# The first chunk's probabilities: transposed by products with a scaled diagonal instead of being scaled first

## Chip, cores and metric

One core of one Trainium2 chip. The metric is the device time of one execution in microseconds; beside it stands the span of the profiled execution, from its first to its last instruction. Lower is better.

## What is computed

Top-k attention followed by two feed-forward layers, all in fp32. There are 4 batches, 8 heads, 576 positions, head width 64, 2304 tokens in all; the feed-forward layers go 512 to 2048 to 512.

```python
scores = scale * np.matmul(q, k.transpose(0, 1, 3, 2))
kth = np.partition(scores, -top_k, axis=-1)[..., -top_k:-top_k + 1]      # top_k = 32
scores = np.where(scores >= kth, scores, -1000000000.0)
scores = scores - np.max(scores, axis=-1, keepdims=True)
attn = np.exp(scores)
attn = attn / (np.sum(attn, axis=-1, keepdims=True) + 1e-09)
out = np.matmul(attn, v)
...
x = out as [2304, 512]
x = max(0.01 * h, h) @ w_out,          h = x @ w_in      # first layer
x = curve(h) @ w2_out,                 h = x @ w2_in     # second layer
```

## The kernel before

**Items and tiles.** Attention is cut into 80 items (`ITEMS`). An item is up to 128 rows of one pair of heads: two tiles of 128 rows by 576 scores, one for each head (a few "mixed" items hold the last 64 rows of both heads in one tile). 144 tiles in all. Four head pairs with the same rows make a chunk's input: chunk 0 is batch 0, rows 0 to 255, that is items 0 to 7, tiles 0 to 15 (`starts_early(it.gp)` is true for just these). There are seven chunks (`CHUNKS`).

**Steps.** All engines follow one written-out order of steps s = 0, 1, 2, ..., each engine with its own in-order list of instructions and semaphores between them. `score_step` says in which step an item's scores are made, `exp_tile` which tile's exponential stands in a step, `out_step` when an item is transposed: items 0 to 7 go out in steps 6, 8, 10, ..., 20. `make_plan` fills the steps from 21 on (`READY[0]`) with units of the feed-forward layers; before step 21 there are none, apart from the first three units' products over three quarters of the input, which stand just ahead of item 7's transposes in step 20.

**An item's way.** TensorE makes the scores (L923, L924) in PSUM; ScalarE copies them scaled to SBUF (L1102, L1109). VectorE finds the 32 largest of each row with four MAX8 (L1304) and three MATCH_REPLACE8 (L1308) a tile, some 5 us a tile. ScalarE's `keep` (L1128, L1130) masks by the 32nd value, `exponential` (L1138) makes the probabilities in `probs` and their row sums. VectorE closes the sum (`close_sum`, L1315) and inverts it (`invert_sum`, L1320). Then `normalise` multiplies the probabilities by it, in place: the first head's 576 columns on ScalarE (L1144), the second head's on GpSimd (L798), for item 7 on VectorE (L1325). TensorE's `transpose` turns them in nine transposes with the identity (L939, L945, and L946 for the last 64 columns of both heads at once). ScalarE copies them to `p_t` and `p_rem` (`copy_transposed`, L1151, L1152), one step after the transposes. After two items of a head pair TensorE multiplies with the values (L962), ScalarE copies the result as the chunk's input (L1172, L1174), GpSimd makes its low half (L804).

**ScalarE's order in a step before 21**: `normalise` of the item that goes out, `copy_transposed` of the one before, `copy_values`, `keep`, score copies, `exponential`, weight pieces. **TensorE's**: scores, values, transposes, scores that are spilled.

**Spilled scores.** Items 22 to 27 get their scores in steps 7, 9, 11, 13, 17 and 18 (`SPILLED_AT`), long before their turn. ScalarE copies them into one of three stages (`stages`: the buffers `part_r`, `part_o` and `y_acc`, which are not yet in use), SyncE stores them to DRAM (L685) and loads them again later (L692). The first hidden unit (`read_bank`, `u.h == 0`) waits for the last store of each stage.

**Feed-forward.** A unit is 128 output rows of a layer's half: products with weights split in a high and a low part (L1003, L1004, L1011). Weights come through `raw`, are split by ScalarE (L1088, L1079) and GpSimd (L792, L785, L781).

Of the kernel before, what the change touches and what calls it, by code (L numbers as in the profile page):

```python
# [8 lines left out]
ALU = mybir.AluOpType  # L9
ACT = mybir.ActivationFunctionType  # L10

P = 128
B, H, S, D = 4, 8, 576, 64
# [6 lines left out]
KC = S // P  # L20
MAIN = KC * P
REST = S - MAIN
# [64 lines left out]
T_SLOTS = 4  # L87
# [128 lines left out]
def starts_early(gp):  # L216

    return gp <= CHUNKS[0].last_gp
# [29 lines left out]
FIRST_LATE = min(it.n for it in ITEMS if it.first > READY[0] + 2)  # L248
SPILLED_AT = {22: 7, 23: 9, 24: 11, 25: 13, 26: 17, 27: 18}
SPILLED = list(SPILLED_AT)  # L250
STAGES = 3


def score_step(it):
# [258 lines left out]
def by_pool(it):  # L513

    return it.gp <= CHUNKS[1].last_gp and not it.mixed and it.last != FIRST_END and not sooner(it)


def by_dve(it):
    return not it.mixed and not by_pool(it)


def scaled(kind, it):

    return sum(kind(o) for o in ITEMS[:it.n + 1])


def need(eng, sem, value):
    if value > 0:
        eng.wait_ge(sem, value)


def build(nc, kqd, vd, wd, out_t):
# [3 lines left out]
    with ExitStack() as ctx:  # L536
        def sb(name, shape, dt=F32):
            return ctx.enter_context(nc.sbuf_tensor(name, shape, dt))

        def ps(name, shape):  # L540
            return ctx.enter_context(nc.psum_tensor(name, shape, F32))

        def sem(name):
            return ctx.enter_context(nc.semaphore(name))
# [11 lines left out]
        row_inv = sb("row_inv", [P, T_SLOTS, 2])  # L556
# [3 lines left out]
        ident = sb("ident", [P, P])  # L560

        gate = sb("gate", [P, 2, GATE_COLS], F32R)
        part_r = sb("part_r", [P, G_SLOTS, WIDE])
        part_o = sb("part_o", [P, G_SLOTS, WIDE])
        y_acc = sb("y_acc", [P, CK, WIDE])
# [2 lines left out]

        raw = sb("raw", [P, RAW_SLOTS, PIECE])
        later = xy[:, 1, :, :, :].rearrange("p h c n -> p (h c n)")  # L570
        stages = [part_r[:, :, :].rearrange("p a n -> p (a n)"), part_o[:, :, :].rearrange("p a n -> p (a n)"),
                  y_acc[:, :, :].rearrange("p a n -> p (a n)")]
        stages = [a[:, 0:2 * S].rearrange("p (h n) -> p h n", h=2) for a in stages]
        split = later[:, 0:SPLIT_SLOTS * 2 * PIECE].rearrange("p (a h n) -> p a h n", a=SPLIT_SLOTS, h=2)

        ps_s = ps("ps_s", [P, 2, 512])
        ps_t = ps("ps_t", [P, 2 * KC, P])
        ps_av = ps("ps_av", [P, 512])
        ps_f = ps("ps_f", [P, BANKS, 512])
        ps_rem = ps_av[:, WIDTH:WIDTH + P]  # L580
# [11 lines left out]
        out_stored = sem("out_stored")  # L592
        spill_stored = [sem("spill_stored%d" % a) for a in range(STAGES)]
        spill_loaded = [sem("spill_loaded%d" % a) for a in range(S_SLOTS)]

        zeroed = sem("zeroed")
        ident_ready = sem("ident_ready")
# [11 lines left out]
        probs_ready = sem("probs_ready")  # L609
        probs_ready_pool = sem("probs_ready_pool")  # L610
        probs_ready_dve = sem("probs_ready_dve")
        transposed = sem("transposed")
# [19 lines left out]

        def spilled(it, where):
            return where[:, 0:it.tiles, :]

        def x_parts(gp):


            b, g = divmod(gp // PAIRS, 2)
            first = g * GROUP_WIDTH[0]  # L640
            buf, pair, width = xy[:, b % 2, :, :, :], gp % PAIRS, GROUP_WIDTH[g]
            if b < B - 1:
                spans = [(first, 0, width)]
            elif g == 0:
                spans = [(WIDE, 0, S - WIDE), (0, S - WIDE, width - S + WIDE)]
            else:
                spans = [(first + WIDE - S, 0, width)]
            return [(buf[:, 0, pair, to:to + n], buf[:, 1, pair, to:to + n], slice(at, at + n)) for to, at, n in spans]
# [22 lines left out]
        def _(sp):  # L671
# [10 lines left out]
            def store_spilled(it):  # L682
                a = SPILL_ORDER.index(it.n)
                sp.wait_ge(scores_copied, 2 * PLACE[it.n] + 2)
                sp.dma_start(spilled(it, s_dram[a, :, :, :]),  # L685
                             spilled(it, stages[a % STAGES])).then_inc(spill_stored[a % STAGES], 16)

            def load_spilled(it):
                a = SPILL_ORDER.index(it.n)
                sp.wait_ge(spill_stored[a % STAGES], 16 * (a // STAGES + 1))  # L690
                sp.wait_ge(kept, ITEMS[it.n - S_SLOTS].last + 1)
                sp.dma_start(spilled(it, scores[:, it.n % S_SLOTS, :, :]),  # L692
                             spilled(it, s_dram[a, :, :, :])).then_inc(spill_loaded[it.n % S_SLOTS], 16)
# [75 lines left out]
        def _(pool):  # L769
# [24 lines left out]

            def normalise(it):
                pool.wait_ge(inv_ready, it.n + 1)
                p = probs[:, it.n % P_SLOTS, S:2 * S]
                pool.tensor_tensor(p, p, row_inv[:, it.n % T_SLOTS, 1:2].to_broadcast([P, S]),  # L798
                                   ALU.mult).then_inc(probs_ready_pool, 1)
# [62 lines left out]
            for s, (first, second, third) in enumerate(PLAN):  # L862
                if s < READY[0] and s in OUT_AT and by_pool(OUT_AT[s]):
                    normalise(OUT_AT[s])
                if s >= READY[0] and s + 1 in OUT_AT and by_pool(OUT_AT[s + 1]):
                    normalise(OUT_AT[s + 1])
# [28 lines left out]
        def _(pe):  # L895
# [31 lines left out]
            def transpose(it):  # L927
                pe.wait_ge(probs_ready, it.n + 1)
                if by_pool(it):
                    pe.wait_ge(probs_ready_pool, scaled(by_pool, it))  # L930
                elif by_dve(it):
                    pe.wait_ge(probs_ready_dve, scaled(by_dve, it))
                if ITEMS_SCORED[it.n] > SCORED_EARLY:
                    pe.wait_ge(scores_copied, 2 * ITEMS_SCORED[it.n])
                need(pe, p_t_copied, it.n)
                need(pe, x_copied, it.gp)
                p = probs[:, it.n % P_SLOTS, :]
                for c in range(KC):
                    pe.transpose(ps_t[:, c, :], p[:, c * P:(c + 1) * P], ident[:, :])  # L939
                if it.mixed:  # L940
                    pe.transpose(ps_t[:, KC, :], p[:, S - P:S], ident[:, :])
                    pe.transpose(ps_rem[0:REST, :], p[:, MAIN:S], ident[:, :]).then_inc(transposed, 1)
                    return
                for c in range(KC):
                    pe.transpose(ps_t[:, KC + c, :], p[:, S + REST + c * P:S + REST + (c + 1) * P], ident[:, :])  # L945
                pe.transpose(ps_rem, p[:, MAIN:MAIN + P], ident[:, :]).then_inc(transposed, 1)  # L946
# [89 lines left out]
            for s, (first, second, third) in enumerate(PLAN):  # L1036
                if s < READY[0]:
                    for it in SCORED_AT[s]:
                        score(it)
                    if s - 1 in VALUES_AT:  # L1040
                        values(VALUES_AT[s - 1])
                    if s == READY[0] - 1:
                        pe.wait_ge(top_ready, FIRST_END + 1)
                        for u in EARLY_UNITS:
                            begin(u)
                    if s in OUT_AT:
                        transpose(OUT_AT[s])
                    for it in SPILL_AT[s]:
                        score(it)
                    if s == READY[0] - 1:  # L1050
                        values(VALUES_AT[s])
                    continue
# [12 lines left out]
                if s in OUT_AT:  # L1065
                    transpose(OUT_AT[s])
# [6 lines left out]
        def _(act):  # L1073
# [17 lines left out]
            def copy_scores(it):  # L1091
                k = PLACE[it.n]
                dst = scores[:, it.n % S_SLOTS, :, :]
                if it.n in SPILLED_AT:
                    a = SPILL_ORDER.index(it.n)
                    dst = stages[a % STAGES]
                    need(act, spill_stored[a % STAGES], 16 * (a // STAGES))
                if k == 0:
# [41 lines left out]

            def normalise(it):
                act.wait_ge(inv_ready, it.n + 1)
                p = probs[:, it.n % P_SLOTS, 0:S]
                act.activation(p, p, ACT.Copy, scale=row_inv[:, it.n % T_SLOTS, 0:1]).then_inc(probs_ready, 1)  # L1144

# [30 lines left out]
            def read_bank(u):  # L1176
# [13 lines left out]
                if u.h == 0:  # L1190
                    for a in range(min(STAGES, len(SPILLED))):
                        act.wait_ge(spill_stored[a], 16 * len(range(a, len(SPILLED), STAGES)))
# [37 lines left out]
            for s, (first, second, third) in enumerate(PLAN):  # L1230
# [41 lines left out]
                if done and sooner(done):  # L1272
                    normalise(done)
                if s + 1 in OUT_AT and not sooner(OUT_AT[s + 1]):
                    normalise(OUT_AT[s + 1])
# [20 lines left out]
        def _(dve):  # L1296
# [24 lines left out]

            def normalise(it):
                dve.wait_ge(inv_ready, it.n + 1)
                p = probs[:, it.n % P_SLOTS, S:2 * S]
                dve.tensor_scalar(p, p, row_inv[:, it.n % T_SLOTS, 1:2], None, ALU.mult).then_inc(probs_ready_dve, 1)  # L1325

# [62 lines left out]
            for s in range(-VECTOR_AHEAD, len(PLAN)):  # L1389
# [15 lines left out]
                if new:  # L1405
                    it = ITEM_OF[t]
# [104 lines left out]
```

## Time and profile before

| | |
|---|---|
| median of three runs | 1159.14 us (1154.64 to 1160.17) |
| profiled execution | 1157.35 us, its span 1155.5 us |
| TensorE, products | 1090.2 us busy (94%) |
| VectorE | 870.8 us (75%) |
| ScalarE | 779.5 us (67%) |
| GpSimd | 477.3 us (41%) |
| mean granted TensorE clock | 0.984 of full |

The busy shares are averages over a head, in which the first chunk's attention is made, a middle, in which attention and feed-forward run side by side, and a long rest. The profile says for each instruction when it started, how long it took, and what ended the idle time of its engine before it. The granted clock is 1.00 at 2.4 GHz and 0.50 at 1.2 GHz. A group of equal instructions in a row is merged into one line of the timeline (x4), and its duration includes the last one's tail.

### The profile page before, as it was taken

To read this page: it belongs to the slowest core of one execution; us is meant where nothing else is said; L and a number is where in the kernel's file an instruction comes from. 1 tells how busy PE (TensorE), PEld (TensorE's weight loads), DVE (VectorE), ACT (ScalarE), POOL (GpSimd) and SP (SyncE) were. 2 spreads that over 40 slices of the span, in tenths; PEclk is the share of its full clock that TensorE was granted. 3 is DMA by queue.
4 is the path that set the end of the run, shared out by engine and by line. 5 is a ranking of instruction groups with operands and counts; after the bars stand their busy time and mean duration, and the time that the engine had idled before them with its cause. 6 is when DMAs were issued, how large, how long until landed. Compare 5 with 4: busy or idle time off the path is not lost.

```text
span 1155.5 us, 21187 instructions
## 1 busy us (share of the span) xinstructions
PE 1090.2 (94%) x7544; PEld 1003.5 (87%) x7544; DVE 870.8 (75%) x1914; ACT 779.5 (67%) x1804; POOL 477.3 (41%) x514
## 2 busy tenths in 40 slices
PE   5467998999999999999999999999999999999998
PEld 3246887799989999999998879998899999999998
DVE  7999978999999898999979979988994005300234
ACT  6777879876698777887779858678785224322332
POOL 5864659552363332642236324134441134222322
PEclk9889999999999999999999989999999999999999
DMA  7998988988667787888766757656456577787774
GB/s 236 374 400 324 400 311 312 360 333 311 234 206 262 248 308 281 291 293 289 240 231 235 244 182 242 215 194 205 148 188 228 203 253 254 256 297 246 256 247 137
DMA packets 92407, 302.59 MB, mean 262 GB/s; under 512 B 10256, under 2 KB 13968, under 8 KB 92304
## 3 DMA queue, kind: packets, MB, share of 16 engines
q1 hardware_dynamic: 88272, 296.52, 73.0%
q10 hardware_dynamic: 4032, 4.72, 1.1%
q8 instruction: 61, 1.00, 0.3%
q14 instruction: 42, 0.34, 0.1%
HBM read 259.39 MB, written 41.81 MB: 261 GB/s over the span
## 4 chain that ended last, share of the span: by engine, by line
PE 79%; DVE 9%; ACT 8%; issue 2%; POOL 2%; DMA 0%; POOLq 0%; SPq 0%; ACTq 0%; DVEq 0%
PE ps_f L1003 21%; PE ps_f L1011 21%; PE ps_f L1004 20%; PE ps_av L962 6%; DVE top L1304 4%; PE ps_s L923 3%; DVE work L1308 3%; PE ps_t L939 2%; PE ps_t L945 2%; PE ps_t L923 1%; ACT probs L1138 1%; ACT probs L1130 1%; DVE part_r L1331 1%; POOL gate L813 1%; PE ps_t L924 1%
## 5 line engine op out<-in xcount | busy, mean ns | idle before, releaser
L1304 DVE MAX8 top<-work 128x8 f32<-128x576 f32 x432 | 310.8, 745 | 0.2
L1003 PE MATMUL ps_f<-xy,w_ring 128*128 128x384 f32 (+2 forms) x896 | 288.2, 322 | 4.5 <-ACT part_o L1196 1.9
L1003 PE MATMUL ps_f<-gate,w_ring 128*128 128x384 f32 (+2 forms) x896 | 286.2, 319 | 0.0
L1011 PE MATMUL ps_f<-gate,w_ring 128*128 128x384 f32 (+2 forms) x896 | 281.2, 314 | 2.8 <-POOL gate L813 2.7
L1011 PE MATMUL ps_f<-xy,w_ring 128*128 128x384 f32 (+2 forms) x896 | 280.6, 313 | 1.9 <-POOL xy L804 1.2
L1004 PE MATMUL ps_f<-gate,w_ring 128*128 128x384 f32 (+2 forms) x896 | 280.6, 313 | 0.0
L1004 PE MATMUL ps_f<-xy,w_ring 128*128 128x384 f32 (+2 forms) x896 | 280.0, 313 | 0.0
L1308 DVE MATCH_REPLACE8 work<-top,work 128x576 f32<-128x576 f32 x288 | 213.7, 742 | 0.0
L813 POOL TENSOR_TENSOR gate<-part_r,gate 128x384 fp32r<-128x384 f32 (+2 forms) x112 | 101.1, 903 | 241.1 <-ACT gate L1200 240.7
L1003 PEld LDWEIGHTS ps_f<-xy,w_ring 128*128 128x128 f32 x896 | 169.4, 189 | 17.2 <-issue 11.3
L1003 PEld LDWEIGHTS ps_f<-gate,w_ring 128*128 128x128 f32 x896 | 170.0, 190 | 6.9 <-issue 6.3
L1339 DVE TENSOR_TENSOR y_acc<-ps_f,y_acc 128x384 f32<-128x384 f32 (+2 forms) x56 | 27.7, 494 | 195.7 <-PE ps_f L1011 195.6
L1011 PEld LDWEIGHTS ps_f<-gate,w_ring 128*128 128x128 f32 x896 | 169.9, 190 | 4.1 <-POOL gate L813 4.1
L1011 PEld LDWEIGHTS ps_f<-xy,w_ring 128*128 128x128 f32 x896 | 169.3, 189 | 3.0 <-POOL xy L804 1.7
L1004 PEld LDWEIGHTS ps_f<-gate,w_ring 128*128 128x128 f32 x896 | 170.2, 190 | 0.0
L1004 PEld LDWEIGHTS ps_f<-xy,w_ring 128*128 128x128 f32 x896 | 169.6, 189 | 0.0
L813 POOL TENSOR_TENSOR gate<-part_o,gate 128x384 fp32r<-128x384 f32 (+2 forms) x112 | 103.1, 922 | 80.2 <-ACT gate L1208 80.1
L1331 DVE SCALAR_TENSOR_TENSOR part_r<-part_r 128x384 f32<-128x384 f32 (+2 forms) x112 | 70.0, 625 | 64.9 <-ACT part_o L1196 64.8
L1138 ACT ACTIVATE probs<-probs,shift 128x576 f32<-128x576 f32 x144 | 113.1, 785 | 0.8
L1304 DVE MAX8 top<-scores 128x8 f32<-128x576 f32 x144 | 108.0, 750 | 6.8 <-ACT scores L1102 6.8
L1130 ACT ACTIVATE probs<-scores,top 128x576 f32<-128x576 f32 x144 | 112.6, 782 | 0.0
L1308 DVE MATCH_REPLACE8 work<-top,scores 128x576 f32<-128x576 f32 x144 | 106.8, 742 | 0.0
(92 smaller groups left out, 1833.7 us busy)
## 6 DMA issues: line engine op xcount, KB each, us to landing
w_ring<-w_split SPq DMA_DIRECT2D x408, 512.0 KB, 4.3
w_split<-w_ring SPq DMA_DIRECT2D x40, 512.0 KB, 6.5
raw<-wd SPq DMA_DIRECT2D x64, 256.0 KB, 6.2
w_split<-xy SPq DMA_DIRECT2D x24, 512.0 KB, 6.3
v_sb<-vd SPq DMA_DIRECT2D x32, 320.0 KB, 6.1
kq<-kqd SPq DMA_DIRECT2D x16, 480.0 KB, 4.7
kq<-kqd SPq DMA_DIRECT2D x15, 416.0 KB, 5.3
scores<-s_spilled SPq DMA_DIRECT2D x6, 576.0 KB, 7.4
```

The lines of the kernel that those rows point to most:

```text
L813: pool.tensor_tensor(gate_of(u, 1), src[:, u.h % G_SLOTS, 0:u.width], gate_of(u, 0).bitcast(F32), ALU.subtract).then_inc(gate_low_done[u.l ...
L923: pe.matmul(out[:, 0, 0:PART], q[0:D, rows[0]], k[0:D, even:even + PART], start=start, stop=stop)
L962: mm = pe.matmul(ps_av[a * D:(a + 1) * D, 0:width], w, x, start=c == 0, stop=c == KC)
L1003: pe.matmul(out, w[:, 0, m], high, start=first, stop=False)
L1004: pe.matmul(out, w[:, 1, m], high, start=False, stop=False)
L1011: mm = pe.matmul(out, w[:, 0, m], low, start=False, stop=end)
L1130: act.activation(probs[:, it.n % P_SLOTS, a * S:(a + 1) * S], scores[:, it.n % S_SLOTS, a, :], ACT.Prelu, bias=last, scale=-1.0, alpha=1.0 ...
L1138: act.activation(p, p, ACT.Exp, bias=shift[:, t % TOP_SLOTS:t % TOP_SLOTS + 1], scale=-STEEP, accum_out=row_sum[:, it.n % T_SLOTS, a:a + 1 ...
L1304: op = dve.max(top[:, t % TOP_SLOTS, 8 * r:8 * r + 8], source(t, r))
L1308: dve.match_replace(work[:, t % 2, :], top[:, t % TOP_SLOTS, 8 * r:8 * r + 8], source(t, r), LOWEST).then_inc(dve_step, 1)
L1331: dve.scalar_tensor_tensor(out=r, in0=r, scalar=1.0, in1=r, op0=ALU.min, op1=ALU.mult).then_inc(curved, 1)
L1339: dve.tensor_tensor(y_cols(u), bank(u), y_cols(u), ALU.add).then_inc(read_by_dve, 1)
```

## The change

For the eight items of the first chunk `normalise` no longer touches the probabilities. It writes a diagonal matrix of 128 by 128 instead, the identity with each row multiplied by that row's reciprocal sum: one for the first head (ScalarE) and one for the second (GpSimd; VectorE for item 7). `transpose` then multiplies: probabilities as weights, diagonal as the moving operand, which transposes and scales at once. These are ordinary fp32 products, not transposes: eight of 128 by 128, and two for the last 64 columns of each head, whose results go to the two halves of `ps_rem`. Four items' diagonals have room (`DIAGS`), and they lie in `y_acc`. So the spill has two stages left, `part_r` and `part_o` (`STAGES = 2`). All other items are scaled and transposed as before.

```diff
--- before.py
+++ after.py
@@ -248,7 +248,8 @@
 FIRST_LATE = min(it.n for it in ITEMS if it.first > READY[0] + 2)
 SPILLED_AT = {22: 7, 23: 9, 24: 11, 25: 13, 26: 17, 27: 18}
 SPILLED = list(SPILLED_AT)
-STAGES = 3
+STAGES = 2
+DIAGS = 4
 
 
 def score_step(it):
@@ -568,9 +569,10 @@
 
         raw = sb("raw", [P, RAW_SLOTS, PIECE])
         later = xy[:, 1, :, :, :].rearrange("p h c n -> p (h c n)")
-        stages = [part_r[:, :, :].rearrange("p a n -> p (a n)"), part_o[:, :, :].rearrange("p a n -> p (a n)"),
-                  y_acc[:, :, :].rearrange("p a n -> p (a n)")]
+        stages = [part_r[:, :, :].rearrange("p a n -> p (a n)"), part_o[:, :, :].rearrange("p a n -> p (a n)")]
         stages = [a[:, 0:2 * S].rearrange("p (h n) -> p h n", h=2) for a in stages]
+        diag = y_acc[:, :, :].rearrange("p a n -> p (a n)")[:, 0:DIAGS * 2 * P]
+        diag = diag.rearrange("p (s h n) -> p s h n", s=DIAGS, h=2)
         split = later[:, 0:SPLIT_SLOTS * 2 * PIECE].rearrange("p (a h n) -> p a h n", a=SPLIT_SLOTS, h=2)
 
         ps_s = ps("ps_s", [P, 2, 512])
@@ -632,6 +634,9 @@
 
         def spilled(it, where):
             return where[:, 0:it.tiles, :]
+
+        def scale_of(it, a):
+            return diag[:, it.n % DIAGS, a, :]
 
         def x_parts(gp):
 
@@ -794,6 +799,11 @@
 
             def normalise(it):
                 pool.wait_ge(inv_ready, it.n + 1)
+                if starts_early(it.gp):
+                    need(pool, transposed, it.n - DIAGS + 1)
+                    pool.tensor_tensor(scale_of(it, 1), ident[:, :], row_inv[:, it.n % T_SLOTS, 1:2].to_broadcast([P, P]),
+                                       ALU.mult).then_inc(probs_ready_pool, 1)
+                    return
                 p = probs[:, it.n % P_SLOTS, S:2 * S]
                 pool.tensor_tensor(p, p, row_inv[:, it.n % T_SLOTS, 1:2].to_broadcast([P, S]),
                                    ALU.mult).then_inc(probs_ready_pool, 1)
@@ -935,6 +945,16 @@
                 need(pe, p_t_copied, it.n)
                 need(pe, x_copied, it.gp)
                 p = probs[:, it.n % P_SLOTS, :]
+                if starts_early(it.gp):
+                    for a in range(2):
+                        for c in range(KC):
+                            at = a * (S + REST) + c * P
+                            pe.matmul(ps_t[:, a * KC + c, :], p[:, at:at + P], scale_of(it, a), start=True, stop=True)
+                    for a in range(2):
+                        mm = pe.matmul(ps_rem[a * D:(a + 1) * D, :], p[:, MAIN + a * REST:MAIN + (a + 1) * REST],
+                                       scale_of(it, a), start=True, stop=True)
+                    mm.then_inc(transposed, 1)
+                    return
                 for c in range(KC):
                     pe.transpose(ps_t[:, c, :], p[:, c * P:(c + 1) * P], ident[:, :])
                 if it.mixed:
@@ -1140,6 +1160,12 @@
 
             def normalise(it):
                 act.wait_ge(inv_ready, it.n + 1)
+                if starts_early(it.gp):
+                    need(act, ident_ready, it.n == 0)
+                    need(act, transposed, it.n - DIAGS + 1)
+                    act.activation(scale_of(it, 0), ident[:, :], ACT.Copy,
+                                   scale=row_inv[:, it.n % T_SLOTS, 0:1]).then_inc(probs_ready, 1)
+                    return
                 p = probs[:, it.n % P_SLOTS, 0:S]
                 act.activation(p, p, ACT.Copy, scale=row_inv[:, it.n % T_SLOTS, 0:1]).then_inc(probs_ready, 1)
 
@@ -1321,6 +1347,12 @@
 
             def normalise(it):
                 dve.wait_ge(inv_ready, it.n + 1)
+                if starts_early(it.gp):
+                    dve.wait_ge(ident_ready, 1)
+                    need(dve, transposed, it.n - DIAGS + 1)
+                    dve.tensor_scalar(scale_of(it, 1), ident[:, :], row_inv[:, it.n % T_SLOTS, 1:2], None,
+                                      ALU.mult).then_inc(probs_ready_dve, 1)
+                    return
                 p = probs[:, it.n % P_SLOTS, S:2 * S]
                 dve.tensor_scalar(p, p, row_inv[:, it.n % T_SLOTS, 1:2], None, ALU.mult).then_inc(probs_ready_dve, 1)
```

## Rows read from the trace of the kernel before

**Rows 1.** Busy time by stretch of the span: us, each engine (instructions), granted clock, DMA share, GB/s.
```profile
24.00:103.00 79.00, 47.08 (x291) 32.61 (x287) 73.81 (x171) 59.29 (x123) 50.58 (x53) 0.85 0.95 358
103.00:240.00 137.00, 126.06 (x971) 111.85 (x971) 122.98 (x278) 118.64 (x295) 95.23 (x101) 0.99 0.93 339
240.00:1156.00 916.00, 904.29 (x6244) 851.83 (x6243) 657.87 (x1432) 586.55 (x1359) 320.83 (x347) 0.99 0.70 242
```

**Rows 2.** Timeline of VectorE: start us, us, line; in brackets the idle before it.
```profile
44.02 0.21 DVE L1315 TENSOR_SCALAR row_eps<-row_sum 128x1 f32<-128x1 f32 x2 [0.84 <-ACT probs L1138]
...
76.19 0.21 DVE L1315 TENSOR_SCALAR row_eps<-row_sum 128x1 f32<-128x1 f32 x2 [1.65 <-ACT probs L1138]
...
94.79 0.22 DVE L1315 TENSOR_SCALAR row_eps<-row_sum 128x1 f32<-128x1 f32 x2 [1.69 <-ACT probs L1138]
```

**Rows 3.** Timeline of ScalarE, first chunk's items.
```profile
34.25 0.78 ACT L1144 ACTIVATE probs<-probs,row_inv 128x576 f32<-128x576 f32 x1 [1.56 <-DVE row_inv L1320]
34.93 0.28 ACT L1128 ACTIVATE shift<-top 128x1 f32<-128x1 f32 x1
...
41.98 0.27 ACT L1152 ACTIVATE p_rem<-ps_av 128x128 f32<-128x128 f32 x1
42.13 0.29 ACT L1128 ACTIVATE shift<-top 128x1 f32<-128x1 f32 x1
...
51.02 1.02 ACT L1151 ACTIVATE p_t<-ps_t 128x1024 f32<-128x1024 f32 x1
...
56.50 0.63 ACT L1109 ACTIVATE y_acc<-ps_s 128x576 f32<-128x576 f32 x1
...
90.88 1.03 ACT L1151 ACTIVATE p_t<-ps_t 128x1024 f32<-128x1024 f32 x1
```

**Rows 4.** Groups of instructions, 0 to 330 us, shapes apart: busy us, mean ns, idle before.
```profile
L798 POOL TENSOR_TENSOR probs<-probs,row_inv 128x576 f32<-128x576 f32 x14 | 16.1, 1147 | 20.3 <-DVE row_inv L1320 20.3
...
L1325 DVE TENSOR_SCALAR probs<-probs,row_inv 128x576 f32<-128x576 f32 x10 | 7.1, 711 | 0.4
```

**Rows 5.** Timeline of TensorE, 30 to 140 us.
```profile
42.39 1.95 PE L962 MATMUL ps_av<-p_t,v_sb 128*64 128x256 f32 x16 [1.37 <-ACT p_rem L1152]
...
48.71 0.40 PE L923 MATMUL ps_s<-kq 64*128 64x288 f32 x1
...
48.95 0.40 PE L923 MATMUL ps_f<-kq 64*128 64x288 f32 x1
...
50.49 0.27 PE L946 MATMUL ps_av<-ident,probs 128*128 128x128 f32 x1
...
88.46 1.09 PE L939 MATMUL ps_t<-ident,probs 128*128 128x128 f32 x4 [2.39 <-ACT x_raw L1174]
...
90.19 0.42 PE L946 MATMUL ps_av<-ident,probs 128*128 128x128 f32 x1
...
97.41 0.60 PE L939 MATMUL ps_t<-ident,probs 128*128 128x128 f32 x4
97.85 0.60 PE L945 MATMUL ps_t<-ident,probs 128*128 128x128 f32 x4
```

**Rows 6.** Timeline of TensorE, scores from rounded halves.
```profile
331.55 0.29 PE L923 MATMUL ps_s<-kq_split 64*128 64x288 f32 x1
...
331.68 0.29 PE L923 MATMUL ps_s<-kq_split 64*128 64x288 f32 x1
```

**Rows 7.** Waits of ScalarE, 24 to 103 us: total, times, longest.
```profile
ACT p_t L1151 <- PE ps_av L946: 3.5, 4, 2.6
```

**Rows 8.** Busy time of TensorE in a half microsecond.
```profile
88.00:88.50 0.50, 0.04 (x1) 0.78 1.04 426
```

**Rows 9.** Timeline of TensorE, item 8.
```profile
119.07 1.08 PE L939 MATMUL ps_t<-ident,probs 128*128 128x128 f32 x4 [2.05 <-issue]
```

**Rows 10.** The spill's DRAM tensor: issues by source, and time to landing.
```profile
L685 SPq DMA_DIRECT2D s_spilled<-part_r x2: 489/753/1017, 41.1 to 73.3; - x2
...
DMA to landing us min/median/max: 5.2/7.0/11.3
```

## The prediction

> **What bounds the kernel now.** I read the busy times by stretch first, then each engine's timeline in the head, then the waits. Three stretches differ [rows 1]. From 240 us on TensorE is busy 904.29 of 916 us, so whatever moves its work there moves the end one for one. From 24 to 103 us (the first chunk's attention) TensorE is busy 47.08 of 79 us and VectorE 73.81: VectorE's top-32 search paces the head and stands still for 5.2 us only. Between 103 and 240 us both are about nine tenths busy and run in step. The change works in the head, so what counts is (a) whether VectorE's standstills get longer or shorter, and (b) when TensorE can begin the first chunk's feed-forward products.
>
> VectorE stands still where it closes an item's sum and ScalarE's exponential is late: 0.84 us, 1.65 us and 1.69 us in three of the places [rows 2]. Between two of them ScalarE runs one fixed round: scale the item that goes out, keep, copy scores, exponential, copy the previous transposes, keep, exponential. So a round gets longer when TensorE's transposes end later than ScalarE comes to copy them, and shorter by what the scaling saves. Savings before item 1 are lost: ScalarE waits 1.56 us for VectorE there [rows 3].
>
> **ScalarE, VectorE, GpSimd.** The scaling of 576 columns holds ScalarE for 34.93 - 34.25 = 0.68 us; the new scaling of 128 columns is nearest to the 128-column copy, 42.13 - 41.98 = 0.15 us [rows 3]. That is 0.53 us less a round; bounds 0.4 (by its whole 0.27 us) and 0.55. GpSimd's 1.15 us scaling [rows 4] becomes something between nothing and 1.15; by columns 0.26, and I take 0.4. It is the releaser of the transposes only for items 0 and 5. VectorE's one scaling (item 7; 0.71 us mean, 0.4 us where it stands here) becomes 0.1: VectorE gains 0.3 us once [rows 4].
>
> **TensorE.** An item had nine transposes. Four of them start 97.85 - 97.41 = 0.44 us apart from the next four: 0.11 us each at the full clock. At the lower one four last 1.09 us with a tail of 0.42 for the last: (1.09 - 0.42) / 3 = 0.22 us each [rows 5]. The new form is eight full fp32 products of 128 moving columns and two with 64-column weights. No such product is in the trace; its price comes from its neighbours. A full fp32 product is two instructions: the eight value products over the main columns are sixteen [rows 5]. One such instruction streams 288 columns in 48.95 - 48.71 = 0.24 us [rows 5], where one on rounded halves takes 331.68 - 331.55 = 0.13 us [rows 6]; fp32 thus costs two cycles a column, and 128 columns take 128 x 0.24 / 288 = 0.107 us, just the price of a transpose. So a product is two transposes' worth. The two 64-wide ones go to different column halves, as the value products do, whose sixteen instructions of 256 columns end after 1.95 us, half of what 256 x 0.24 / 288 x 16 = 3.4 us would be one after the other [rows 5]: together 0.21 us. New sum 18 x 0.11 = 1.98 us against 0.99: **+0.99 us an item at the full clock, +1.98 at the lower**. Bounds: nothing (if a 128-column pass cost half of this), and +2.97 (below).
>
> The Trainium skill (TensorE: Matmul & The Clock Gate, Terms) says that transpose mode is four times faster for fp32. By that rule the item would cost 4 x 0.99 = 3.96 us, +2.97 at the full clock. The rows above, two cycles a column and two instructions, give twice, and I sum by them; the rule is a rival below.
>
> **Round by round.** ScalarE waited for the transposes in four of eight rounds, 3.5 us in all, 2.6 of them in the last [rows 7]; so items 1, 3 and 5 already wait 0.2 to 0.4 us. A round changes by (added TensorE time) - 0.53 - (slack).
> - Item 0: absorbed in the 1.56 us wait.
> - Item 1: no slack; the clock rises midway in its transposes. With 7 of 18 slots slow where most of the old ones were slow too: +0.5 us.
> - Item 2: the last transpose ends at 50.49 + 0.27 = 50.76 and the copy starts at 51.02 [rows 3, 5]: slack 0.26. 0.99 - 0.53 - 0.26 = +0.2.
> - Item 3: like item 1, +0.4.
> - Item 4: no wait there; the whole saving counts, -0.5.
> - Item 5: the transposes end later, but ScalarE has to wait for the next top 32 anyway: 0.
> - Item 6: starts at 88.46 after 2.39 us without work, just as the granted clock falls (0.78 in that half microsecond) [rows 5, 8]. The old ones end at 90.19 + 0.42 = 90.61 and the copy starts at 90.88: slack 0.27 [rows 3, 5]. TensorE's work before it now ends later and this item starts a little sooner, so the pause is about 1.9 us. If the clock holds, 1.98 us full is what 1.98 us slow was: -0.5. If it falls: 1.98 - 0.53 - 0.27 = +1.2, less some slots after the clock's rise, +0.8.
> Sum for VectorE: 0.5 + 0.2 + 0.4 - 0.5 + 0 - 0.5 = +0.1 us, or +1.4 with the slow item 6; minus 0.3 once for item 7.
> - Item 7: its scaling is hidden behind the first products of three units; its transposes start when these end (97.41 [rows 5]), so scaling less buys nothing and the feed-forward starts 0.99 us later.
> What is late next is item 8: TensorE stands 2.05 us before its transposes at 119.07, waiting for VectorE's chain, and restarts at the lower clock (1.08 us for four) [rows 9]. The 1.0 us goes into that pause. With a pause of 1 us instead of 2 the clock may hold, which gives back at least 9 x 0.11 = 1.0 us.
> **Total**: from -1.0 (clock holds at items 6 and 8) to +2.4 (holds at neither, all late); I take +0.1.
>
> **The two stages.** Spilled scores now wait for the store two spills earlier instead of three. The tightest case is the third one: its copy starts at 56.50 [rows 3], the store whose buffer it would now reuse is issued at 41.1 and the slowest store lands after 11.3 us [rows 10], so by 52.4. 4.1 us to spare: nothing. If that cover were gone, ScalarE's copy and with it keep and the exponential would stand behind the wait, one for one. The first unit still waits for the last two stores, as before. The new wait for a free diagonal (four items back) is fulfilled a whole round earlier.
>
> **Against the measure.** The profiled execution took 1157.35 us (span 1155.5), 1.8 below the median 1159.14. +0.1 on it is 1157.45; beside the median, 1159.2. Half a per cent, 5.8 us, is about what a measurement of this kernel can tell from no change.
>
> **Rivals.**
> - Forecast, gains and losses cancel (-2 to +3 us): chance 0.74.
> - Warmer clock: the products close TensorE's pauses, and every cold stretch of the head goes. Items 1 and 3 then end sooner than now (1.98 full against 1.6 to 1.8 part slow, less 0.53: -0.3 each), 2 +0.2, 4 -0.5, 6 -0.5, 8 -1.0: -2.4, 1156.7 us. For it: two of the falls come just at the end of a 2 us pause. Against: the pauses before items 1 and 3 are longer. Chance 0.10 (within 0.5%).
> - Slower, by the clock: it stays low in every round once transposes are 3.96 us. +1.4 in items 1 and 3, +1.2 in item 2 and after a lead of late rounds 1.2 in item 4, 6 alike, 5 +0.4: about +7, and item 7 adds 2: +9, 1168 us. It decides from three slow rounds on. Against: in every busy stretch of the head the clock rose. Chance 0.06.
> - Slower, by price: each product costs four transposes (+2.97). Rounds 1, 2, 3: 2.97 - 0.53 - slack = 2.4, 2.2, 2.4; item 4 about 1.4; 5 1.2; 6 1.2; 7 3.0, of which 2.05 goes into item 8's pause: about +12, 1171 us. Against: rows 5 and 6. Chance 0.06.
> - More than half a per cent gained: VectorE's 5.2 us of standstill in the head [rows 1] are all that this change can reach there, so it would need these and item 8's pause: 0.04.
>
> **How the numbers follow.** Slower by over 0.5%: the two slow rivals, 0.12. Faster: 0.04, and 0.02 for a shift of phase later on. The rest, 0.82, within. The range takes in both neighbours of the forecast and a median's scatter (before: 1154.64 to 1160.17): 1153.5 to 1165.0.
>
> **What the profile after would show.** ScalarE's 128-column scaling at 0.15 us spacing; sixteen instructions in about 1.7 us per item at the full clock; transposed copies that wait in items 1, 2, 3; sum-closing waits of VectorE with about the same total as 5.2 us; no wait on a spill store; item 8 with a shorter pause. Wrong would be: products over 0.15 us an instruction, low clock through the whole head, or TensorE's pauses after 103 us growing by more than 2 us.

## The result: 0.23% slower, with larger terms inside than were forecast

The changed kernel takes 1160.59 us (median of 20 runs, 1159.25 to 1161.94), the kernel before 1158.18 us (20 runs, 1154.64 to 1160.17). The ratio is 1.0023, 95% interval 1.0016 to 1.003: a loss of 2.7 us, clear of the scatter and within the half per cent that was forecast. The profiled execution has a span of 1158.3 us against 1155.5.

Busy time of the changed kernel by stretch, in the columns of [rows 1] (us, TensorE, its weight loads, VectorE, ScalarE, GpSimd, granted clock, DMA share, GB/s):

```profile
24.00:103.00 79.00, 54.25 (x342) 40.29 (x341) 68.58 (x161) 54.30 (x117) 45.28 (x53) 0.87 0.92 336
103.00:240.00 137.00, 125.34 (x980) 110.05 (x979) 125.72 (x284) 117.55 (x291) 91.96 (x98) 1.00 0.93 347
240.00:1156.00 916.00, 906.40 (x6271) 854.22 (x6269) 660.88 (x1437) 590.19 (x1369) 324.40 (x350) 1.00 0.70 242
```

In the head TensorE works 7.2 us more than before (54.25 against 47.08) and VectorE gets 5.2 us less done (68.58 against 73.81 [rows 1]). These are the places where VectorE now stands still before it closes a sum, the counterparts of [rows 2] and two more (start us, us, line; in brackets the wait before it and what ended it). The first line is from the kernel before, the counterpart of 70.01:

```profile
64.63 0.21 DVE L1315 TENSOR_SCALAR row_eps<-row_sum 128x1 f32<-128x1 f32 x2 [0.73 <-ACT probs L1138]
...
46.28 0.21 DVE L1341 TENSOR_SCALAR row_eps<-row_sum 128x1 f32<-128x1 f32 x2 [3.14 <-ACT probs L1158]
...
56.88 0.21 DVE L1341 TENSOR_SCALAR row_eps<-row_sum 128x1 f32<-128x1 f32 x2 [0.69 <-ACT probs L1158]
...
70.01 0.21 DVE L1341 TENSOR_SCALAR row_eps<-row_sum 128x1 f32<-128x1 f32 x2 [3.22 <-ACT probs L1158]
...
81.45 0.21 DVE L1341 TENSOR_SCALAR row_eps<-row_sum 128x1 f32<-128x1 f32 x2 [1.52 <-ACT probs L1158]
...
99.69 0.21 DVE L1341 TENSOR_SCALAR row_eps<-row_sum 128x1 f32<-128x1 f32 x2 [1.33 <-ACT probs L1158]
```

The five waits are 9.9 us, where the four of the kernel before (0.84, 0.73, 1.65, 1.69) were 4.9. Against the kernel before, the closing that follows item 1's transposes is 2.26 us late (46.28 for 44.02), the one behind item 3's has added 2.5 us more, those behind items 2, 4 and 6 move by +0.6, -0.1 and -0.4. The last closing of the chunk is 99.69 for 94.79 [rows 2]: 4.9 us late. The transposes themselves, first two lines of the kernel before (the score product behind item 2's transposes, and item 7's last transpose), then the changed kernel:

```profile
50.70 0.51 PE L923 MATMUL ps_s<-kq 64*128 64x288 f32 x1
...
98.28 0.27 PE L946 MATMUL ps_av<-ident,probs 128*128 128x128 f32 x1
...
39.17 3.73 PE L952 MATMUL ps_t<-y_acc,probs 128*128 128x128 f32 x16
42.83 0.44 PE L954 MATMUL ps_av<-y_acc,probs 128*64 128x128 f32 x4
...
51.45 2.05 PE L952 MATMUL ps_t<-y_acc,probs 128*128 128x128 f32 x16
53.43 0.44 PE L954 MATMUL ps_av<-y_acc,probs 128*64 128x128 f32 x4
53.80 0.51 PE L933 MATMUL ps_s<-kq 64*128 64x288 f32 x1
...
62.83 3.78 PE L952 MATMUL ps_t<-y_acc,probs 128*128 128x128 f32 x16
...
102.30 1.95 PE L952 MATMUL ps_t<-y_acc,probs 128*128 128x128 f32 x16
104.17 0.44 PE L954 MATMUL ps_av<-y_acc,probs 128*64 128x128 f32 x4
```

The price at the full clock is a little above the one worked out: sixteen instructions from 51.45 to 53.43 are 0.124 us each, in item 7 (102.30 to 104.17) 0.117 us, forecast 0.11, and the two 64-wide products take 0.37 us (53.43 to 53.80) for 0.21. A whole item 7 lasts 2.31 us (102.30 to the end of the last line) where its nine transposes lasted 1.14 (97.41 to 98.55): +1.17 us, forecast +0.99. In item 2 it is 2.35 us up to the next score product for 1.14 (49.56 to 50.70 before). But items 1 and 3 ran all but wholly at the lower clock, 3.66 us from 39.17 to 42.83 for sixteen instructions. The granted clock (the column behind TensorE's busy time) says why:

```profile
40.50:41.00 0.50, 0.50 (x4) 0.50 1.05 426
42.50:43.00 0.50, 0.50 (x7) 0.79 0.87 305
60.00:60.50 0.50, 0.00 (x0) 0.50 1.10 447
66.00:66.50 0.50, 0.50 (x3) 0.50 0.99 388
66.50:67.00 0.50, 0.49 (x5) 0.90 1.05 424
```

TensorE restarted at 36.95 us, and the clock rose in the half microsecond from 42.5; before it was back at 40.5. For item 3 it restarted at 60.61 and got the full clock in the one from 66.5, when the products were through; before, it restarted at 57.71 and had the full clock from 61.0. Why the clock rose later, with TensorE busy from the restart on in both kernels, no run isolates. Item 0's sixteen instructions lasted as long (3.68 us from 24.98 to 28.66), which cost nothing: the closing behind them is at 33.24 us, before at 33.28. (The column reads 1.00 there, up to 32 us; these durations show the lower clock.)

ScalarE waited for the transposes:

```profile
ACT p_t L1177 <- PE ps_av L954: 9.3, 6, 2.7
ACT y_acc L1166 <- DVE row_inv L1346: 7.1, 8, 1.0
ACT scores L1129 <- PE ps_s L934: 3.8, 3, 1.4
ACT shift L1148 <- DVE top L1330: 1.0, 4, 0.3
```

The first row answers to [rows 7], but for item 7, whose wait of 4.1 us (2.6 before) now falls behind 103 us. Without item 7 it is 9.3 us in six waits, where it was 0.9 us in three. The last row is why the shorter scaling bought so little. ScalarE's scaling and what follows it, in two rounds:

```profile
34.21 0.40 ACT L1166 ACTIVATE y_acc<-ident,row_inv 128x128 f32<-128x128 f32 x1 [1.02 <-DVE row_inv L1346]
34.86 0.29 ACT L1148 ACTIVATE shift<-top 128x1 f32<-128x1 f32 x1 [0.26 <-DVE top L1330]
...
47.26 0.40 ACT L1166 ACTIVATE y_acc<-ident,row_inv 128x128 f32<-128x128 f32 x1 [1.01 <-DVE row_inv L1346]
47.57 0.36 ACT L1198 ACTIVATE xy<-ps_av 128x256 fp32r<-128x256 f32 x1
```

Where `copy_values` follows (47.26 to 47.57) the scaling now holds ScalarE for 0.31 us, not the 0.15 forecast. Where `keep` follows (34.21 to 34.86), ScalarE waits 0.26 us for the MAX8 that VectorE runs right after the reciprocal; the scaling of 576 columns had just covered that MAX8, 0.68 us [rows 3] against 0.65 now. In four of the eight rounds the saving is 0.03 us.

Then most of the lateness is given back. The first feed-forward product starts at 108.80 us for 102.74, 6.1 us late, but item 8's transposes, the counterpart of [rows 9], come after a pause of 0.95 us instead of 2.05, at the full clock (the lines at 102.74 and 131.63 are the kernel before):

```profile
102.74 0.39 PE L1003 MATMUL ps_f<-xy,w_ring 128*128 128x256 f32 x1 [0.47 <-ACT xy L1172]
108.80 0.39 PE L1023 MATMUL ps_f<-xy,w_ring 128*128 128x256 f32 x1 [0.47 <-ACT xy L1198]
...
124.04 0.63 PE L959 MATMUL ps_t<-ident,probs 128*128 128x128 f32 x4 [0.95 <-issue]
...
131.63 0.60 PE L939 MATMUL ps_t<-ident,probs 128*128 128x128 f32 x4
135.04 0.60 PE L959 MATMUL ps_t<-ident,probs 128*128 128x128 f32 x4
```

They are 4.97 us late (124.04 for 119.07) and, at 0.63 us for four instead of 1.08, start a stretch in which TensorE no longer runs at 0.50: item 9's transposes (135.04 for 131.63) are 3.41 us late, and so, within 0.03 us, are the later ones up to 300 us. The span ends 2.8 us later, so the last 0.6 us come back behind that.

### The profile page after: what moved, and what is told of

Read it like the earlier page. It is cut to its first block, busy times and chain, and to the rows that moved or that the text cites. A ratio compares the mean times of both kernels' runs of the same rounds, so it can differ in the third digit from the quotient of the medians.

```text
span 1158.3 us, 21372 instructions
## 1 busy us (share of the span) xinstructions
PE 1098.8 (95%) x7632; PEld 1011.8 (87%) x7632; DVE 871.4 (75%) x1914; ACT 777.1 (67%) x1804; POOL 472.3 (41%) x514
## 4 chain that ended last, share of the span: by engine, by line
PE 80%; DVE 8%; ACT 7%; issue 3%; POOL 2%; DMA 0%; POOLq 0%; SPq 0%; ACTq 0%; DVEq 0%
PE ps_f L1023 21%; PE ps_f L1031 21%; PE ps_f L1024 20%; PE ps_av L982 6%; DVE top L1330 4%; PE ps_s L933 3%; DVE work L1334 2%; PE ps_t L959 2%; PE ps_t L965 2%; PE ps_t L952 1%; PE ps_t L933 1%; DVE part_r L1363 1%; ACT probs L1150 1%; ACT probs L1158 1%; POOL gate L823 1%
```

## The experiments

Every ratio is to the kernel before, timed beside it on the same chip. Three groups share such runs: e1 to e4, e5 to e8, and e9 to e11. Each interval reaches about 0.1% to either side.

**Undoing parts.** The first three take one part of the change each, the fourth leaves it whole and holds the clock. The cuts are shortened.

```diff
 e1_two_stages (from the kernel before)
-STAGES = 3
+STAGES = 2

 e2_products_only (from the kernel before)
+if starts_early(it.gp):
+    pe.matmul(ps_t[:, a * KC + c, :], p[:, at:at + P], ident[:, :], ...)   # 8 and 2, as in the change

 e3_scaling_only (from the changed kernel, in transpose)
-if starts_early(it.gp):
+if False:
```

> The kernel before with two stages for the spilled scores and nothing else. Theory A (the loss sits in TensorE's longer transposes): no wait appears on a stage's store, since the tightest reuse had 4 us to spare, and the time is that of before, within 0.05%. Rival (the stages cost): ScalarE's copy of a spilled item waits for a store, and some or all of the 2.4 us are here (+0.1 to +0.2%).

Measured: 0.9996 (0.9985 to 1.0006). No store of a stage shows among ScalarE's waits from 24 to 103 us. The stages are not the cause.

> The kernel before, its probabilities scaled in place as ever, but the first chunk's items transposed by full fp32 products with the identity. Only the added TensorE work is left of the change. Theory A: all of the loss is here, +0.2 to +0.3%, with VectorE's sum-closing standstills up from 5.9 to about 11 us, and at most 0.5 us more than the changed kernel, since the shorter scaling was worth little. Rival (savings and costs of like size, as forecast): the savings of 0.53 us a round are missing now, so it ends 2 us or more above the changed kernel, +0.4% or more.

Measured: **1.0053** (1.0041 to 1.0065), 6.1 us. This is within the rival's range (+0.4% or more) and above theory A's: the products alone cost twice the whole change, 6.1 - 2.7 = 3.4 us more. Not all of that is missing savings. In this kernel item 2's products, which the changed kernel ran at the full clock (2.05 us), met the lower one as well:

```profile
51.74 3.58 PE L942 MATMUL ps_t<-ident,probs 128*128 128x128 f32 x16
```

> The changed kernel with its diagonals written, two stages, but nine plain transposes with the identity, so the first chunk's probabilities stay unscaled: the division by the sum is left out for it. Only the savings are left. Theory A: in items 0, 1, 3 and 5 ScalarE gets its 0.3 us back only to wait for VectorE's fourth MAX8, so little comes out: 0 to -1 us (-0.09%). Rival (forecast): 0.53 us in most rounds, about -2.2 us (-0.19%).

Measured: 0.9985 (0.9975 to 0.9994), a gain of 1.7 us, between the two (0 to 1 and 2.2), and with an interval (0.7 to 2.9 us) that reaches both. This kernel leaves out the division by the sum for the first chunk. Products alone and savings alone add to 4.4 us where the change measures 2.7; the intervals do not tell these two apart.

> The changed kernel with idle products of the identity with itself, into a PSUM bank not yet in use, put into TensorE's pauses ahead of the scores of items 22, 7, 8, 9, 10 and the transposes of items 5 and 6 (5, 8, 5, 20, 5, 16 and 3 of them, 0.21 us each at the full clock). Theory A with the clock as its larger half: the granted clock stays full through items 1 and 3, whose sixteen instructions take 2.0 instead of 3.75 us, VectorE's standstills fall from 10.8 to about 7 us, and the feed-forward starts 3 to 4 us sooner; the end comes 1.5 to 3 us sooner than the changed kernel's, at or just under the time before (0.999 to 1.001). Rival (the number of products, not the clock): nothing gained, 1.002 or more because the filling delays the scores.

```diff
 e4_products_warm (from the changed kernel)
+FILL_SCORE = {22: 5, 7: 8, 8: 5, 9: 20, 10: 5}
+FILL_TRANSPOSE = {5: 16, 6: 3}
+def fill(n):
+    for _ in range(n):
+        pe.matmul(ps_f[:, 2, 0:P], ident[:, :], ident[:, :], start=True, stop=True)
 def score(it):
+    fill(FILL_SCORE.get(it.n, 0))
 def transpose(it):
+    fill(FILL_TRANSPOSE.get(it.n, 0))
```

Measured: **0.9976** (0.9967 to 0.9985): with idle work added, the changed kernel beats the kernel before by 2.8 us. That is 5.4 us from the changed kernel's own ratio, more than theory A's 1.5 to 3. Item 1's transposes and VectorE's closings behind items 1 and 3 in it:

```profile
38.15 2.05 PE L960 MATMUL ps_t<-y_acc,probs 128*128 128x128 f32 x16
40.13 0.44 PE L962 MATMUL ps_av<-y_acc,probs 128*64 128x128 f32 x4
```

```profile
43.59 0.21 DVE L1349 TENSOR_SCALAR row_eps<-row_sum 128x1 f32<-128x1 f32 x2 [0.41 <-ACT probs L1166]
...
64.52 0.21 DVE L1349 TENSOR_SCALAR row_eps<-row_sum 128x1 f32<-128x1 f32 x2 [0.42 <-ACT probs L1166]
...
94.20 0.22 DVE L1349 TENSOR_SCALAR row_eps<-row_sum 128x1 f32<-128x1 f32 x2 [1.33 <-ACT probs L1166]
```

The sixteen instructions take 1.98 us, not 3.66. The standstills are 0.41 and 0.42 us instead of 3.14 and 3.22, and the last closing is at 94.20 us, sooner than before the change (94.79). So the clock carries the larger half of the head's loss, as theory A said. How much the idle products would give the kernel before is the next question. (In this profile the clock still fell once, from 94.6 to 98.0 us.)

**Which items, and the kernel before with its clock held.**

```diff
 e6_items_1_3, e7_items_2_4_6, e8_items_4_6_warm (from the changed kernel, in all four places)
-if starts_early(it.gp):
+if it.n in DIAG_ITEMS:      # (1, 3), (2, 4, 6), (4, 6)

 e5_before_warm, e8_items_4_6_warm: fill() as above with these numbers, and ahead of the first three units
+FILL_SCORE = {22: 5, 7: 11, 8: 7, 9: 20, 10: 7}
+FILL_TRANSPOSE = {5: 20, 6: 5}
+fill(6)
```

> The kernel before (scaled in place, plain transposes, three stages) with idle products in TensorE's pauses: ahead of the scores of items 22, 7, 8, 9, 10, of the transposes of items 5 and 6, and of the first units (5, 11, 7, 20, 7, 20, 5 and 6 of them). If the clock's fall in the pauses of the head is a cost of its own, in either form of the transposes, this gains over before: items 1 and 3 end some 1 us sooner, the first units run at the full clock: 0.997 to 0.999. If it mattered only to the products, nothing: 1.000.

Measured: **0.9970** (0.9960 to 0.9981), 3.5 us faster than the kernel before. With the full clock from 30 us on, ScalarE waits for no transposes but item 7's (24 to 103 us), and of VectorE's standstills before a closing only two are left after 30 us:

```profile
74.53 0.21 DVE L1324 TENSOR_SCALAR row_eps<-row_sum 128x1 f32<-128x1 f32 x2 [1.66 <-ACT probs L1147]
...
93.14 0.22 DVE L1324 TENSOR_SCALAR row_eps<-row_sum 128x1 f32<-128x1 f32 x2 [1.70 <-ACT probs L1147]
```

> The changed kernel with diagonals and products for items 1 and 3 only; the other six are scaled and transposed as before. Theory A (the loss is made where ScalarE already waited for the transposes and the clock was low): VectorE's standstills before the sums of the next items rise by 2 us and more each, as in the changed kernel, and the end is 1.002 to 1.004. Rival (each item costs alike): a quarter of the change, 1.0006.

Measured: 1.0036 (1.0024 to 1.0048), theory A's range; the rival's 1.0006 is out. Two items' products cost at least as much as all eight (1.0016 to 1.003; the intervals overlap). Both closings behind them:

```profile
46.23 0.21 DVE L1342 TENSOR_SCALAR row_eps<-row_sum 128x1 f32<-128x1 f32 x2 [2.68 <-ACT probs L1159]
...
69.39 0.21 DVE L1342 TENSOR_SCALAR row_eps<-row_sum 128x1 f32<-128x1 f32 x2 [3.28 <-ACT probs L1159]
```

Moreover, nothing is given back at item 8: the pause before it is 2.06 us there, the clock falls at its transposes (0.59 in the half microsecond from 124.0), and item 9's transposes, at 136.46 us, are 4.8 us late, as much as the first feed-forward product (107.52 for 102.74). In the changed kernel item 7's longer transposes had narrowed that pause.

> The changed kernel with diagonals and products for items 2, 4 and 6 only, the rounds in which ScalarE copies the values' result right behind the scaling and the saving is not waited away. Theory A: +0.2 to +0.6, -0.3 and 0 us: 0.999 to 1.0005. Rival (each item costs alike): 1.0009 or more.

Measured: 1.0013 (1.0002 to 1.0024). The value lies in the rival's range (1.0009 or more) and above theory A's upper end, which the interval still takes in. Its trace shows more than a cost per item: the last closing is at 99.63 us, as late as the changed kernel's, and here it is item 2 that meets the lower clock, which in the changed kernel had the full one.

```profile
56.76 0.21 DVE L1342 TENSOR_SCALAR row_eps<-row_sum 128x1 f32<-128x1 f32 x2 [2.27 <-ACT probs L1159]
```

```profile
50.00:51.00 1.00, 1.00 (x5) 0.50 1.04 420
...
52.00:53.00 1.00, 1.00 (x12) 1.00 1.04 408
```

Item 6's sixteen instructions start at 92.06 us and take 2.93 us, the clock falling 0.8 us after their start. Item 3 has plain transposes here, and yet the clock stays low around them from 58.8 to 69.0 us; the value products behind them then hold up ScalarE by 0.71 us.

Which items are hit thus depends on where the clock's falls come to lie, and any shift in the head moves them. "Items 1 and 3" is right for the profiled execution; as a rule for where products are cheap it fell.

> Products for items 4 and 6 only, and the idle products of the warmed kernel before. Both parts where they should help: 0.996 to 0.998, 0 to 1 us under the warmed kernel before. If it is not under that one, the product form buys nothing even at its best places.

Measured: 0.9968 (0.9958 to 0.9978), the same as e5_before_warm within the intervals. Of the kernels that leave nothing out it is the fastest, by a margin over e5 that is not resolved (medians 1154.39 and 1155.07 us). So whether products buy anything even at their best places stays open. In its profile the clock fell at item 8, at 116.6 us.

**Price and saving with the clock held.** Three more kernels complete a square: the change, its products alone and its scaling alone, each with the idle products of e5. Their clock is not held everywhere: in all of them item 0 still meets the lower one, before the first idle products, and in e11's profile the clock fell once more, from 33.1 to 36.5 us, mostly under idle products.

> The whole change with the same idle products as the warmed kernel before. With the clock held, products cost 0.99 us an item and the first feed-forward product comes 1 us after item 7's; the pause of 2 us before item 8 takes this up. Theory A (at the full clock price and saving are of one size, the loss was the clock): within 1 us of the warmed kernel before, 0.9965 to 0.9985 of before. Rival (products cost by their number too): as far above the warmed before as the change is above before, 0.9993 or more.

> Scaled in place as before, transposed by products with the identity, with the same idle products: only the price of the products, at the full clock. Theory A: in the warmed kernel before, ScalarE waits for no transposes but the last, so part of the 0.99 us an item is covered; 1 to 3 us over it: 0.998 to 1.0. The same form without them was 1.0053. Rival (the number, not the clock): 1.002 and more.

> Diagonals written and plain transposes with the identity, with the same idle products; the first chunk's probabilities stay unscaled. Only the saving, with the clock held. Theory A: most of the saving is waited away for VectorE's MAX8; 0 to 1.5 us under the warmed kernel before: 0.9957 to 0.997.

| ratio to before | as it is | clock held |
|---|---|---|
| scaled in place, transposes (before) | 1 | 0.9970 (0.9960 to 0.9981) |
| products alone | 1.0053 (1.0041 to 1.0065) | 0.9987 (0.9977 to 0.9997) |
| scaling alone (first chunk's division left out) | 0.9985 (0.9975 to 0.9994) | 0.9958 (0.9943 to 0.9973) |
| the change | 1.0023 (1.0016 to 1.003) | 0.9976 (0.9965 to 0.9986) |

All three came out as theory A had them. In the right column the terms add up: products +0.17% (2.0 us), scaling -0.12% (1.4 us), both together +0.06% (0.7 us), which the intervals do not tell from nothing. The top of that column was measured in another group than the rest. Within one group the change lies 1.5 us under the products alone and 1.8 us over the scaling alone (medians 1155.30, 1156.83 and 1153.49 us), which puts the two terms together at +0.3 us. In the left column the products cost 0.53% and the change 0.23%.

Of the loss of 2.7 us, 0.3 to 0.7 us are thus the parts themselves and about 2 us the clock; each of these differences of ratios is known only to some 1.7 us either way. The traces say the same: with the clock held (e9, first line below) the last closing is 1.4 us behind e5's 93.14, without it 4.9 us behind the kernel before. Where the 2.0 us of the products arise can be read in e10:

```profile
94.52 0.21 DVE L1350 TENSOR_SCALAR row_eps<-row_sum 128x1 f32<-128x1 f32 x2 [1.34 <-ACT probs L1167]
...
44.52 0.21 DVE L1334 TENSOR_SCALAR row_eps<-row_sum 128x1 f32<-128x1 f32 x2 [0.43 <-ACT probs L1157]
...
55.50 0.21 DVE L1334 TENSOR_SCALAR row_eps<-row_sum 128x1 f32<-128x1 f32 x2 [1.07 <-ACT probs L1157]
...
77.66 0.21 DVE L1334 TENSOR_SCALAR row_eps<-row_sum 128x1 f32<-128x1 f32 x2 [1.91 <-ACT probs L1157]
...
96.27 0.21 DVE L1334 TENSOR_SCALAR row_eps<-row_sum 128x1 f32<-128x1 f32 x2 [1.71 <-ACT probs L1157]
```

Most rounds cost some tenths, and the last closing is 96.27 us for 93.14 in e5: 3.1 us of the head, of which the pause before item 8 takes a part.

## Why the prediction was right, and where it was not

- **The outcome.** +2.7 us is within the forecast case (-2 to +3 us), the range and "no change within half a per cent". The direction inside it was not forecast (the total was taken as +0.1), and the small sum came from larger terms: +4.9 us in VectorE's chain, where +0.1 was summed, and +6.1 us at the first feed-forward product, 2.7 us of it given back at item 8. That a head 6.1 us late ended inside the forecast case is in part luck: 2.0 us were forecast to be taken up and given back there. The total's two ends also do not treat VectorE's 0.3 us alike: the upper one leaves it out.
- **TensorE's price per item** (+0.99 us at the full clock, +1.98 at the lower one): right in kind, a fifth low. Two instructions a product, each about a transpose: 0.117 to 0.124 us for 0.107. With the two 64-wide products, at 0.37 us for 0.21, an item costs +1.2 us at the full clock (items 2 and 7). At the lower clock an instruction takes 0.229 us for 0.22. The rival of four transposes a product is refuted, and so, for this product, is the Trainium skill's factor of four (TensorE: Matmul & The Clock Gate, Terms): the trace gives two.
- **"Item 1 ... +0.5" and "Item 3 ... +0.4"** are the steps that failed: 2.3 and 2.5 us. The steps assumed that the clock rises at about the time it rose before, midway. It rose some 2 us later in item 1, and the products were twice as many while it was low. e4 shows that this was the clock: with it held the standstills are 0.4 us. The rival "slower, by the clock" had the mechanism; it asked for all rounds, and it was two, with +2.3 and +2.5 us where it had +1.4.
- **ScalarE's saving of 0.53 us a round**: mis-sized twice. The scaling holds ScalarE 0.31 us instead of 0.15, and in four rounds ScalarE waits for the MAX8 instead, so that 0.03 us are left. The forecast counted on 0.53 us in items 1, 2, 3, 4 and 6, 2.65 us; taken alone, the savings measure 1.7 us, and next to the products with the clock held 1.5. The forecast had named only the wait in front of the scaling, not the next one behind it.
- **VectorE's gain of 0.3 us**: did not come. Its 128-column scaling takes 0.29 us behind a new wait of 0.32 us that the profile puts down to its own reciprocal, 0.69 us from the reciprocal's start to the next search step where it was 0.63. The old scaling waited for the same reciprocal without a gap; the new one asks for two more semaphores, both long fulfilled. Whether they are the 0.32 us is not shown.
- **GpSimd's scaling**: 0.40 us, as taken. **The stages**: nothing, as forecast (e1).
- **Item 2**: +0.6 us (forecast +0.2). With the measured sizes the forecast's own sum comes out: 1.21 - 0.37 - 0.26 = +0.58. **Item 4**: -0.1 (-0.5); of the saving of 0.37 us a new wait of 0.28 for the transposes takes most. **Item 6**: -0.4 (-0.5); the clock held, as in the better of its two cases, after a pause of 1.73 us. **Item 7**: 1.2 more for the first products (6.06 against 4.9 us late; forecast 1.0).
- **VectorE's standstills** were to keep their total of about 5.2 us, and sixteen instructions to take 1.7 us; they were 9.9 us, and 1.9 to 2.0 us.
- **Item 8's pause**: right in mechanism and more in size. It went from 2.05 to 0.95 us, the clock held, and 2.65 us came back from the first product's 6.06 us of lateness.

What stays open: how often the clock falls into which item over many executions, since the profile shows one execution of each kernel; and what made it rise later in items 1 and 3. The products need not be it: in e7 TensorE worked on scores and plain transposes from 60.49 to 64.89 us without a pause, and the clock stayed low.

## What to carry to other kernels

When work is moved onto TensorE in a stretch where it has pauses, price it at the lower clock, and read which instructions actually ran at it. A saving on an in-order engine counts only up to that engine's next wait: look at the row behind the shortened one. And where a bank of PSUM is free, idle products in the pauses are worth trying first; here they gave 0.30%, where the change's savings taken alone gave 0.15%.

## What the hardware showed that was not expected

- Holding the clock from 30 to about 100 us alone shortened the kernel by 3.5 us, with some 15 us of useless TensorE work added (61.89 us busy from 24 to 103 us in e5, 47.08 before).
- The clock can fall while TensorE is at work. In the changed kernel item 5's products start at 82.98 us after a pause of 4.3 us, still at the full clock, which falls 0.7 us later (0.67 over the half microsecond from 83.5):

```profile
83.00:83.50 0.50, 0.50 (x5) 1.00 1.02 414
83.50:84.00 0.50, 0.50 (x6) 0.67 1.00 411
84.00:84.50 0.50, 0.50 (x4) 0.50 1.00 401
87.00:87.50 0.50, 0.50 (x6) 0.92 1.07 363
```

- A pause's length alone did not tell whether the clock fell: before item 8 a pause of 2.05 us ended at the lower clock in the kernel before, one of 2.06 us at the full clock in e5.

```profile
117.44 0.63 PE L947 MATMUL ps_t<-ident,probs 128*128 128x128 f32 x4 [2.06 <-issue]
```
